# First two token tiles listed from five tiles, routing inside the first product, and stores of x from SyncE's queue

## The chip, the cores and the metric

One core of a Trainium2 chip runs the program. The metric is device time in microseconds (us), median of 3 runs. Line numbers such as L1570 are lines of the kernel before.

## What is computed

```python
attn = local + summary attention of q, k, v      # B=2, H=8, S=768, D=64; window 16, 24 block summaries
x = attn reshaped to (B, S, 512)
for b, s:                                        # expert layer, E=8 experts, F=1024
    e = argmax(x @ w_gate) if s == 0 or gate < 0.5 else expert of token s-1
    out[b, s] = p[e] * (relu(x[b, s] @ w1[e]) @ w2[e])
theta = out @ w_theta                            # third layer
y = w_tok_r @ (out*cos(theta)) + w_tok_i @ (out*sin(theta))
u = out + y;  result = u + relu(u @ w_ch)
```

A token's expert depends on the tokens before it in its batch, so the routing is a running maximum over all tokens. With the inputs that the reference draws, 363 tokens of the first batch go to expert 0, and 269 of them are among its first 640 tokens (five tiles of 128).

## The kernel before

**Attention.** The 1536 tokens are 12 tiles of 128, six to a batch (`TPB = 6`, `NT = 12`). TensorE's turn of one tile g (`tile`, in the block of TensorE) is: scores of tile g+2, transposes of p (the exponentials) of tile g, logits of older tiles, transposes of x of tile g-1, and the product with v (`weigh`). In tiles 0 and 1 the transposes of p stand ahead of the scores. VectorE takes the scores from PSUM (L932), finds the maxima (L938), copies logits (L964) and normalises (`norm`, L959), which writes `x_sb`. ScalarE takes the exponentials (L705) and copies transposed p (L712) and x (L717). GpSimd copies windows of keys (L556) and values (L581 to L585) and the summary rows (`move_rows`, L603) into place, and between them it issues the stores of `x_sb` to the DRAM tensor `xd` (L620), one for each tile. SyncE issues the loads of the first expert's weights, `w1_raw` and `w2_raw`, in four steps each (L485, L488).

**First list.** Expert 0 is the first expert. Which tokens fill its first two slot tiles (`FIRST_TILES = 2`) is found early, from the six tiles of the first batch alone, by the functions `first_...` of VectorE and TensorE (tensors `o_...`, `[P, TPB]` wide). `first_list` ends it: it writes two columns of `slot_list` (L1062), on which GpSimd gathers slot tile 0 from `xd` (`load_first`, L608) into `xin`. The gather of slot tile 1 follows when slot tile 0 has been transposed (`xTf_ready`).

**Full routing.** When the logits of all 12 tiles are there (`logits_back`), VectorE runs one chain of short dependent instructions on tensors `r_...` (L1141 to L1192). TensorE helps it three times: `routing_turn` (L1535), `routing_back` (L1539, L1540) and `routing_ranks` (L1545 to L1547). Then the list of all 21 slot tiles is made by `routing_list` (L1554, twelve matmuls, which need `r_ol` of VectorE and `r_ot` of GpSimd, L641), and the rest of `slot_list` is copied (L1198). VectorE afterwards makes the `table` (L1205 to L1224) that tells each slot tile's weights.

**Products.** A slot tile t is gathered, transposed (`transpose_slots`, L1565), copied by ScalarE and VectorE, multiplied with w1 (`product1`), passed through relu, transposed (`transpose_h`, L1592) and multiplied with w2 (`product2`). The products take float32 as two parts: ScalarE rounds a weight step to its high part `w_h` (L756, L786, L792), VectorE subtracts to get the low part `w_l` (`split_step`, L1095), and three matmuls use them (L1570 to L1572). Only the first product of slot tile 0 (L1621) uses unsplit weights. From slot tile 2 on TensorE needs `table_ready`, since it reads from the table where the weights lie.

**Order.** Each engine runs its instructions in the order in which its block lists them, and semaphores order the engines against each other. The queues that matter here are those of SyncE (hardware DMA) and GpSimd (software DMA).

## Time and profile before

| | us |
|---|---|
| median of 3 runs (lowest, highest) | 424.63 (424.21, 425.11) |
| the profiled execution | 423.96 |
| its span in the trace | 422.2 |
| granted clock of TensorE over the span | 0.999 |

The span is the time between the first and last recorded instruction. The profiled execution takes 1.8 us more than its span, and the median lies 0.67 us above the profiled execution. Times of rows count from the start of the span. A row of a timeline gives start, duration, engine, line, operation, the tensors as out<-in, and how often it stands there; matmuls of one row overlap, so that a row's duration is not the sum of its parts. In brackets stands how long the engine sat idle before it, and for whom.

### The profile page before, as it was taken

The numbers are of one execution on the slowest core, as the hardware profiler recorded it, in microseconds if no ns is written. First come the engines' busy times: TensorE is split into PE (matmuls) and PEld (weight loads), VectorE is DVE, ScalarE is ACT, GpSimd is POOL, SyncE is SP. The second block draws the span as 40 slices with busy tenths as digits, with TensorE's granted clock in tenths as the row PEclk, the third lists the DMA queues.
The fourth block names the chain that finished last, engine by engine and source line by source line (L and its number), as shares of the span: only waits on it lengthen the run. The fifth ranks groups of instructions, "written<-read, shape, count | busy, mean of one in ns | idle before, by whom it ended". The sixth has DMA issues, their size and how long they took to land.

```text
span 422.2 us, 8097 instructions
## 1 busy us (share of the span) xinstructions
PE 409.2 (97%) x2791; PEld 328.6 (78%) x2792; DVE 258.0 (61%) x429; ACT 194.1 (46%) x431; POOL 80.8 (19%) x127
## 2 busy tenths in 40 slices
PE   6889999999999999999999999999999999999996
PEld 3668786468888888888888778888888888888885
DVE  4898998898646327363117595666687646454352
ACT  1698995624647326463247464444433143213110
POOL 3697783221112100121110023200000000000000
PEclk9999999999999999999999999999999999999999
DMA  8995551162989933518130025300000000000012
GB/s 293 412 374 170 185 178 78 51 249 73 380 274 397 367 153 90 208 35 338 50 100 26 0 72 202 100 2 0 0 2 0 26 25 0 27 25 27 25 57 93
DMA packets 17424, 54.50 MB, mean 129 GB/s; under 512 B 2033, under 2 KB 2161, under 8 KB 17137
## 3 DMA queue, kind: packets, MB, share of 16 engines
q1 hardware_dynamic: 12560, 40.98, 27.1%
q0 software_dynamic: 2960, 9.70, 7.0%
q10 hardware_dynamic: 1872, 3.41, 2.1%
q8 instruction: 19, 0.31, 0.3%
q14 instruction: 13, 0.10, 0.1%
HBM read 40.46 MB, written 13.63 MB: 128 GB/s over the span
## 4 chain that ended last, share of the span: by engine, by line
PE 77%; DVE 3%; ACT 3%; DVEq 1%; issue 1%; ACTq 0%; POOL 0%
PE ps L1570 15%; PE ps L1572 14%; PE ps L1571 14%; PE ps L1714 8%; PE ps L1715 8%; PE ps L1716 8%; PE ps L1652 2%; PE ps L1592 2%; PE ps L1621 2%; PE ps L1460 2%; ACT w_h L756 1%; PE ps L1565 1%; DVE w_l L1095 1%; PE ps L1432 1%; DVEq L1102 1%
## 5 line engine op out<-in xcount | busy, mean ns | idle before, releaser
L1714 PE MATMUL ps<-z_h,mix_h 128*128 128x512 f32 x144 | 56.9, 395 | 0.0
L1716 PE MATMUL ps<-z_h,mix_l 128*128 128x512 f32 x144 | 56.1, 390 | 0.0
L1715 PE MATMUL ps<-z_l,mix_h 128*128 128x512 f32 x144 | 56.1, 390 | 0.0
L1570 PE MATMUL ps<-w_h,hT_h 128*128 128x512 f32 x104 | 42.0, 404 | 0.8 <-DVE w_l L1095 0.5
L1095 DVE TENSOR_TENSOR w_l<-w_raw,w_h (+1 forms) x32 | 37.4, 1219 | 8.3 <-ACT w_h L756 8.3
L705 ACT ACTIVATE p<-s,nmax 128x120 f32<-128x120 f32 x96 | 36.5, 384 | 11.1 <-DVE nmax L938 11.1
L1572 PE MATMUL ps<-w_l,hT_h 128*128 128x512 f32 x104 | 40.7, 391 | 0.0
L1571 PE MATMUL ps<-w_h,hT_l 128*128 128x512 f32 x104 | 40.5, 390 | 0.0
L1570 PE MATMUL ps<-w_h,xT_h 128*128 128x512 f32 x96 | 38.4, 400 | 0.0
L1571 PE MATMUL ps<-w_h,xT_l 128*128 128x512 f32 x96 | 37.4, 390 | 0.0
L1572 PE MATMUL ps<-w_l,xT_h 128*128 128x512 f32 x96 | 37.4, 390 | 0.0
L841 ACT ACTIVATE ang_a<-ang_c 128x512 f32<-128x512 f32 x12 | 7.6, 632 | 63.6 <-DVE ang_c L1283 63.6
L1119 DVE TENSOR_TENSOR hT_l<-ps,hT_h 128x512 fp32r<-128x512 f32 x26 | 16.7, 684 | 25.6 <-ACT hT_h L770 25.5
L1716 PEld LDWEIGHTS ps<-z_h,mix_l 128*128 128x128 f32 x144 | 27.0, 188 | 5.8
L1714 PEld LDWEIGHTS ps<-z_h,mix_h 128*128 128x128 f32 x144 | 27.0, 188 | 5.4
L1715 PEld LDWEIGHTS ps<-z_l,mix_h 128*128 128x128 f32 x144 | 27.1, 188 | 5.4
L756 ACT ACTIVATE w_h<-w_raw 128x1024 fp32r<-128x1024 f32 x24 | 23.6, 1051 | 7.8 <-PE ps L1572 5.3
L764 ACT ACTIVATE h_sb<-ps 128x1024 f32<-128x1024 f32 x12 | 12.3, 1024 | 29.2 <-PE ps L1572 29.2
L1113 DVE TENSOR_TENSOR xT_l<-ps,xT_h 128x512 fp32r<-128x512 f32 x12 | 8.3, 689 | 28.3 <-ACT xT_h L760 28.3
L1570 PEld LDWEIGHTS ps<-w_h,hT_h 128*128 128x128 f32 x104 | 19.5, 188 | 5.3 <-DVE w_l L1095 1.3
L1572 PEld LDWEIGHTS ps<-w_l,hT_h 128*128 128x128 f32 x104 | 19.5, 188 | 4.4
L1571 PEld LDWEIGHTS ps<-w_h,hT_l 128*128 128x128 f32 x104 | 19.6, 188 | 3.7
(264 smaller groups left out, 860.2 us busy)
## 6 DMA issues: line engine op xcount, KB each, us to landing
w_raw<-w SPq DMA_DIRECT2D x32, 512.0 KB, 6.2
mix_raw<-mix SPq DMA_DIRECT2D x6, 768.0 KB, 6.0
kfull<-k_full SPq DMA_DIRECT2D x8, 400.0 KB, 6.4
q_all<-q_t SPq DMA_DIRECT2D x6, 512.0 KB, 7.3
vpad<-v_pad SPq DMA_DIRECT2D x4, 768.0 KB, 8.8
xd<-x_sb POOLq DMA_DIRECT2D x12, 256.0 KB, 4.6
ys<-y_sb ACTq DMA_DIRECT2D x12, 256.0 KB, 2.0
out<-o SPq DMA_DIRECT2D x12, 256.0 KB, 2.0
```

What stands on the lines that cost most here:

```text
L705: e = act.activation(p_sb[s][:, n // PAIRS, n % PAIRS, :], s_sb[s][:, n, :], ACT.Exp, bias=nmax[s][:, n:n + 1], accum_out=rsum[s][:, n, 0:1])
L756: act.activation(hi[:, i * SW:(i + 1) * SW, :], raw[:, i * SW:(i + 1) * SW, :], ACT.Copy).then_inc(done, 1)
L764: act.activation(h_sb[:, :].rearrange("p (a n) -> p a n", a=2), ps[:, bank:bank + 2, :], ACT.Relu)\
L1095: dve.tensor_tensor(lo[:, bass.ds(i * SW, SW), :], raw[:, bass.ds(i * SW, SW), :], hi[:, bass.ds(i * SW, SW), :].bitcast(f32), ALU.subtrac ...
L1119: dve.tensor_tensor(hT_l[:, c * 4:c * 4 + 4, :], ps[:, B_HT + c, :].rearrange("p (a k) -> p a k", k=P), hT_h[:, c * 4:c * 4 + 4, :].bitcas ...
L1460: pe.matmul(ps[:, B_Y, :], ident, const[:, 0:DM], start=True, stop=True)
L1570: pe.matmul(ps[:, bank, :], a_h[:, k, :], w_h[:, n, :], start=(k == 0), stop=False)
L1571: pe.matmul(ps[:, bank, :], a_l[:, k, :], w_h[:, n, :], start=False, stop=False)
L1572: return pe.matmul(ps[:, bank, :], a_h[:, k, :], w_l[:, n, :], start=False, stop=(k == last))
L1714: pe.matmul(ps[:, i, :], w_h, zh, start=(jb == 0 and m == 0), stop=False)
L1715: pe.matmul(ps[:, i, :], w_h, zl, start=False, stop=False)
L1716: mm = pe.matmul(ps[:, i, :], w_l, zh, start=False, stop=(jb == TPB - 1 and m == 1))
```

## The change

1. The first list is made from five token tiles instead of six (`FROM = TPB - 1`), and each of its steps stands one token tile earlier or more: `first_logits` and `first_maxima` in tile 7 instead of 8, `first_turn` and `first_scan` in tile 9 instead of 10, `first_back` and `first_choice` in tile 10 instead of 11, `first_rank`, `first_ranks`, `first_lanes` and both `first_list` in tile 11, ahead of the last `weigh` and the last `norm`, instead of after them.
2. In tile 10 VectorE copies both halves of transposed p first of all; in tile 11 ScalarE copies both.
3. In tiles 2 and 3 TensorE transposes p ahead of the scores (it did so in tiles 0 and 1 only).
4. SyncE issues the stores of `x_sb`; GpSimd no longer does. GpSimd moves summary rows 2 and 3 after the key and value windows of its first round.
5. `routing_turn`, `routing_back` and `routing_ranks` stand between the matmuls of the first product of slot tile 0, with one filler matmul (`keep_warm`) instead of six ahead of it; `routing_list` stands ahead of the last quarter of `product1(1)` instead of ahead of all of it; the transposes of slot tile 2 stand in the middle of `product2(0)` instead of ahead of it.
6. Four of the eight low parts of the first expert's weights go to GpSimd (`rest`: steps 2 and 3 of w1, 0 and 1 of w2). They stand between the gather of slot tile 1 and `r_ot`. VectorE makes steps 0 and 1 of w1 ahead of `r_scan`, and steps 2 and 3 of w2. VectorE's copy for slot tile 1 (`xT_copy(1)`) moves into the routing chain.
7. ScalarE rounds two steps of w1 ahead of its last copy of transposed x.

```diff
-WARM, WARM_SUM, WARM_SLOTS = (5, 1), (1, 0), (3, 1, 1, 1)
+WARM, WARM_SUM, WARM_SLOTS = (5, 1), (1, 0), 1
+FROM = TPB - 1
@@ SyncE
+            for g in range(NT):
+                sp.wait_ge(norm_done, g + 1)
+                sp.dma_start(xd[g * P:(g + 1) * P, :], x_sb[:, g, :]).then_inc(x0_saved if g < TPB else x_saved, 16)
@@ GpSimd
             for g in range(NT):
-                pool.wait_ge(norm_done, g + 1)
-                pool.dma_start(xd[g * P:(g + 1) * P, :], x_sb[:, g, :]).then_inc(x0_saved if g < TPB else x_saved, 16)
+                if g == NT - 1:
+                    pool.wait_ge(x0_saved, 16 * TPB)
+                    pool.wait_ge(olist_done, 1)
+                    load_first(0)
...
             load_first(1)
+            def rest(i, raw, hi, lo, hi_done, done):
+                pool.wait_ge(hi_done, i + 1)
+                pool.tensor_tensor(lo[:, i * SW:(i + 1) * SW, :], raw[:, i * SW:(i + 1) * SW, :],
+                                   hi[:, i * SW:(i + 1) * SW, :].bitcast(f32), ALU.subtract).then_inc(done, 1)
+            pool.wait_ge(w1_split, STEPS + STEPS // 2)
+            for i in range(STEPS // 2, STEPS):
+                rest(i, w1_raw, w1_h, w1_l, w1_hi, w1_split)
+            for i in range(STEPS // 2):
+                rest(i, w2_raw, w2_h, w2_l, w2_hi, w2_split)
@@ VectorE, tile
+                if g == NT - 2:
+                    pT_copy(g, 0)
+                    pT_copy(g, 1)
+                if g == NT - 1:
+                    first_ranks()
+                    first_lanes()
                 inverse(g, s)
@@ TensorE, tile
-                if sc and g > 1:
+                if sc and g > SUMMARY_TILES:
                     scores(g + 2, s)
+                if g == NT - 1:
+                    first_rank()
                 transpose_p(g, s, first)
@@ TensorE, first product
+                    if (c, k) == (0, 0):
+                        routing_turn()
+                    if (c, k) == (0, 1):
+                        routing_back()
+                    if (c, k) == (1, 0):
+                        routing_ranks()
+                    if (c, k) == (1, 1):
                         transpose_slots(1)
...
-            routing_list()
-            product1(1, 0)
-            transpose_slots(2)
-            product2(0, 0, first=True)
+            product1(1, 0, middle=routing_list)
+            product2(0, 0, first=True, middle=lambda: transpose_slots(2), at=KF // 2)
```

GpSimd's queue after the last value windows, before the change:

```order
L620 DMA xd<-x_sb 128x512 [waits norm_done] x2
L608 DMA xin<-xd,slot_list 128x512 [waits olist_done,x0_saved]
L608 DMA xin<-xd,slot_list 128x512 [waits xTf_ready]
L641 ISA
L641 TENSOR_TENSOR r_ot<-r_in,const 128x252 [waits tiles_ready]
L651 DMA xin<-xd,slot_list 128x512 [waits xTf_ready,list_done,x_saved]
```

and after it, where the instruction that loads GpSimd's code for such operations (ISA) and four subtractions follow the two gathers:

```order
L612 DMA xin<-xd,slot_list 128x512 [waits olist_done,x0_saved]
L612 DMA xin<-xd,slot_list 128x512 [waits xTf_ready]
L648 ISA
L648 TENSOR_TENSOR w_l<-w_raw,w_h 128x1024 [waits w1_hi,w1_split]
L648 TENSOR_TENSOR w_l<-w_raw,w_h 128x1024 [waits w1_hi]
L648 TENSOR_TENSOR w_l<-w_raw,w_h 128x1024 [waits w2_hi] x2
L657 TENSOR_TENSOR r_ot<-r_in,const 128x252 [waits tiles_ready]
L667 DMA xin<-xd,slot_list 128x512 [waits xTf_ready,list_done,x_saved]
```

So `r_ot` now stands behind four more operations of GpSimd.

TensorE from the gather of slot tile 0 (`xin`) to the routing's ranks, before the change (L1460 are fillers, L1621 is the first product):

```order
L1460 MATMUL ps<-const 128x512 x3
L1535 MATMUL ps<-const,r_v 12x128 [waits v_ready]
L1460 MATMUL ps<-const 128x512
L1539 MATMUL ps<-const,r_scan 128x12 [waits scan_ready]
L1540 MATMUL ps<-const,r_scan 128x12
L1460 MATMUL ps<-const 128x512
L1565 MATMUL ps<-const,xin 128x128 [waits xin_in]
L1565 MATMUL ps<-const,xin 128x128 x3
L1460 MATMUL ps<-const 128x512
L1545 MATMUL ps<-r_oe,tri_b 128x96 [waits cum_ready,onehot_ready]
```

and after it (the first product is L1637):

```order
L1585 MATMUL ps<-const,xin 128x128 x3
L1477 MATMUL ps<-const 128x512
L1637 MATMUL ps<-w_raw,xT_f 128x512 [waits w1_in3,w1_in2,xTf_taken,w1_in1,w1_in0]
L1554 MATMUL ps<-const,r_v 12x128 [waits v_ready]
L1637 MATMUL ps<-w_raw,xT_f 128x512
L1558 MATMUL ps<-const,r_scan 128x12 [waits scan_ready]
L1559 MATMUL ps<-const,r_scan 128x12
L1637 MATMUL ps<-w_raw,xT_f 128x512 x3
L1564 MATMUL ps<-r_oe,tri_b 128x96 [waits cum_ready,onehot_ready]
```

The waits for the routing now stand inside the product instead of ahead of it.

VectorE around its last normalisation (`x_sb`), before the change:

```order
L959 TENSOR_TENSOR x_sb<-ps,rinv 128x512 [waits av_ready]
L964 COPY logitsT_164<-ps 128x128 [waits lg_ready]
L1048 SCALAR_TENSOR_TENSOR o_off<-ps,o_oe 128x6 [waits orank_ready]
L1049 TENSOR_SCALAR o_slot<-o_off 128x6 [waits o_link]
L1050 TENSOR_SCALAR o_tile<-o_slot 128x6 [waits o_link]
L1051 TENSOR_SCALAR o_lane<-o_slot 128x6
L1054 TENSOR_TENSOR o_in<-o_tile,const 128x12 [waits o_link]
L1056 TENSOR_TENSOR o_ot<-o_in,const 128x12 [waits o_link]
L1057 TENSOR_TENSOR o_ol<-o_lane,const 128x768
L964 COPY logitsT_165<-ps 128x128 [waits lg_ready]
L1062 CAST slot_list<-ps 128x2 [waits olist_ready]
```

and after it:

```order
L1079 TENSOR_TENSOR o_ol<-o_lane,const 128x640
L968 TENSOR_REDUCE rsafe<-rsum_158 128x8 [waits exp_done]
L970 RECIPROCAL rinv<-rsafe 128x8 [waits rsafe_done]
L981 COPY logitsT_165<-ps 128x128 [waits lg_ready,rinv_done]
L1084 CAST slot_list<-ps 128x2 [waits olist_ready]
L976 TENSOR_TENSOR x_sb<-ps,rinv 128x512 [waits av_ready]
L981 COPY logitsT_164<-ps 128x128 [waits lg_ready]
L1088 TENSOR_TENSOR w_l<-w_raw,w_h 128x1024 [waits w1_hi]
L981 COPY logitsT_165<-ps 128x128 [waits lg_ready]
```

The whole first list now stands ahead of the last normalisation, and the first low part of w1 between the last two copies of logits.

## Rows read from the trace of the kernel before

**Rows 1.** The page: engines' shares, and the chain that ended last by engine.
```profile
PE 409.2 (97%) x2791; PEld 328.6 (78%) x2792; DVE 258.0 (61%) x429; ACT 194.1 (46%) x431; POOL 80.8 (19%) x127
...
PE 77%; DVE 3%; ACT 3%; DVEq 1%; issue 1%; ACTq 0%; POOL 0%
```

**Rows 2.** Timeline of TensorE in the attention tiles (start, us, what, idle before).
```profile
25.32 1.05 PE L1403 MATMUL ps<-kw,q_all 64*64 64x120 f32 x32 [0.69 <-POOL kw L556]
...
28.77 1.15 PE L1432 MATMUL ps<-v,pT 120*64 120x64 f32 x32 [0.43 <-ACT pT L712]
...
58.18 1.05 PE L1403 MATMUL ps<-kw,q_all 64*64 64x120 f32 x32 [0.43 <-POOL kw L556]
...
65.67 1.15 PE L1432 MATMUL ps<-v,pT 120*64 120x64 f32 x32 [0.85 <-DVE pT L943]
```

**Rows 3.** Timeline of TensorE, the list, h and the product of slot tile 2.
```profile
80.39 5.40 PE L1621 MATMUL ps<-w_raw,xT_f 128*128 128x512 f32 x12
...
89.12 0.45 PE L1554 MATMUL ps<-r_ot,r_ol 128*128 128x21 f16 x12
...
100.95 1.03 PE L1592 MATMUL ps<-const,h_sb 128*128 128x128 f32 x8
101.74 0.48 PE L1570 MATMUL ps<-w_h,xT_h 128*128 128x512 f32 x1
```

**Rows 4.** Timeline of VectorE, the routing chain.
```profile
74.17 0.26 DVE L1141 TENSOR_REDUCE r_m<-ps 128x12 f32<-128x96 f32 x1 [0.26 <-PE ps L1455]
...
75.50 1.22 DVE L1095 TENSOR_TENSOR w_l<-w_raw,w_h 128x1024 fp32r<-128x1024 f32 x1
...
78.75 0.58 DVE L1156 TENSOR_TENSOR r_oe<-r_e,const 128x96 bf16<-128x96 int32 x1
79.37 0.36 DVE L1159 TENSOR_TENSOR_SCAN r_cum<-const,r_oe 128x96 bf16<-128x96 f32 x1
79.64 1.20 DVE L1095 TENSOR_TENSOR w_l<-w_raw,w_h 128x1024 fp32r<-128x1024 f32 x1
...
81.93 0.19 DVE L1170 TENSOR_TENSOR_SCAN r_end<-const,r_al 128x16 f32<-128x16 f32 x1
...
82.43 0.20 DVE L1174 TENSOR_TENSOR r_over<-ps,r_al 128x42 f32<-128x42 f32 x1
...
85.11 2.23 DVE L1192 TENSOR_TENSOR r_ol<-r_lane,const 128x768 f16<-128x768 uint32 x2
```

**Rows 5.** Timeline of GpSimd, gathers and its one two-input operation.
```profile
74.64 1.01 POOL L608 DMA_INDIRECT xin<-xd,slot_list  x1 [2.71 <-DVE slot_list L1062]
79.85 1.85 POOL L608 DMA_INDIRECT xin<-xd,slot_list  x1 [4.20 <-PE ps L1565]
85.27 1.25 POOL L641 TENSOR_TENSOR r_ot<-r_in,const 128x252 f16<-128x252 f32 x1 [3.57 <-DVE r_in L1188]
90.53 1.24 POOL L651 DMA_INDIRECT xin<-xd,slot_list  x1 [4.01 <-DVE slot_list L1198]
```

**Rows 6.** The line of the first two gathers: from issue to landing.
```profile
DMA to landing us min/median/max: 3.4/3.9/4.5
```

**Rows 7.** Timeline of all engines: short VectorE operations beside GpSimd's copies.
```profile
60.33 1.04 POOL L603 COPY v<-v 24x1024 f32<-24x1024 f32 x1
...
62.25 0.61 POOL L581 COPY v<-vpad 64x512 f32<-64x512 f32 x1
62.29 0.59 DVE L1020 TENSOR_TENSOR o_t<-o_lg,o_m 128x6 f32<-128x6 f32 x1
```

**Rows 8.** The line of `r_ol`: durations in ns, least, median and greatest.
```profile
L1192 DVE TENSOR_TENSOR r_ol<-r_lane,const x2: 954/1160/1366, 85.1 to 86.0; 128x768 f16<-128x768 uint32 x2
```

**Rows 9.** The line of `r_ot`, the sequencer's instruction ahead of it.
```profile
L641 POOLq MODIFY_POOL_CONFIG  x2: 47/47/47, 81.7 to 81.7; - x2
```

**Rows 10.** Timeline of VectorE, from slot tile 2's copy to the table's last write.
```profile
96.76 0.69 DVE L1113 TENSOR_TENSOR xT_l<-ps,xT_h 128x512 fp32r<-128x512 f32 x1
...
100.46 0.16 DVE L1224 TENSOR_TENSOR table<-r_tf 1x20 int32<-1x20 f32 x1
```

More of the change, by code:

```diff
@@ L479, in _ @@
             load_v(1)
[L480 to L488 removed]
+            for g in range(NT):
+                sp.wait_ge(norm_done, g + 1)
+                sp.dma_start(xd[g * P:(g + 1) * P, :], x_sb[:, g, :]).then_inc(x0_saved if g < TPB else x_saved, 16)
+                if g == 0:
+                    load_q(2)
+                    sp.dma_start(const[:, C_UT:C_END], const_d[:, C_UT:C_END]).then_inc(rconst_in, 16)
+                elif g <= STEPS:
+                    part = slice((g - 1) * SW, g * SW)
+                    sp.dma_start(w1_raw[:, part, :], w1_d[0, :, part, :]).then_inc(w1_in[g - 1], 16)
+                elif g <= 2 * STEPS:
+                    part = slice((g - STEPS - 1) * SW, (g - STEPS) * SW)
+                    sp.dma_start(w2_raw[:, part, :], w2_d[0, :, part, :]).then_inc(w2_in[g - STEPS - 1], 16)
             sp.wait_ge(logits_back, 1)
@@ L615, in _ @@
             value_window(1)
-            for n in range(1, VB):
-                move_rows(0, n)
+            move_rows(0, 1)
             for g in range(NT):
-                pool.wait_ge(norm_done, g + 1)
-                pool.dma_start(xd[g * P:(g + 1) * P, :], x_sb[:, g, :]).then_inc(x0_saved if g < TPB else x_saved, 16)
+                if g == NT - 1:
+                    pool.wait_ge(x0_saved, 16 * TPB)
+                    pool.wait_ge(olist_done, 1)
+                    load_first(0)
                 if g == TPB:
@@ L630, in _ @@
                     value_window(g + 2)
+                if g == 0:
+                    for n in range(2, VB):
+                        move_rows(0, n)
                 if g == TPB - 2:
@@ L986, in tile @@
                     lg_copy(g - 2)
-                if g == TPB + 2:
+                if g == FROM + 2:
                     first_maxima()
-                if g == NT - 3:
+                if g == FROM + 3:
                     first_other()
+                if g == NT - 2:
+                    first_choice()
                 if g == NT - 1:
-                    first_choice()
+                    first_list()
                 norm(g)
-                if g == TPB + 2:
+                if g == FROM + 2:
                     first_fresh()
-                if g == NT - 3:
+                if g == FROM + 3:
                     first_code()
+                    first_keys()
             linked = [0]
@@ L1193, in _ @@
                                   const[:, C_LANE:C_OWN].unsqueeze(1).broadcast_to([P, NT // 2, P]), ALU.is_equal).then_inc(lanes_ready, 1)
-            w1_step(2)
-            xT_copy(1)
             dve.wait_ge(list_ready, 1)
             dve.tensor_copy(slot_list[:, FIRST_TILES:NS], ps[:, B_R, R_LIST + FIRST_TILES:R_LIST + NS]).then_inc(list_done, 1)
-            w1_step(3)
             hT_copy(0)
-            for i in range(STEPS):
+            dve.wait_ge(w2_split, STEPS + STEPS // 2)
+            for i in range(STEPS // 2, STEPS):
                 split_step(i, i, w2_raw, w2_h, w2_l, w2_hi, w2_split)
@@ L1524, in _ @@
             route_logits(NT - 2)
-            first_rank()
             transpose_x(NT - 1)
@@ L1546, in routing_ranks @@
                 pe.matmul(ps[:, B_R, R_RANK:R_RANK + E * NT], ones_b[:, :], r_cum[:, :, :].rearrange("p e j -> p (e j)"), start=False, stop=True)
-                pe.matmul(ps[:, B_R, R_COUNT:R_COUNT + V], ones_b[:, :], r_cum[:, :, TPB - 1:NT:TPB], start=True, stop=True).then_inc(count_ready, 1)
+                pe.matmul(ps[:, B_R, R_COUNT:R_COUNT + V], ones_b[:, :], r_cum[:, :, TPB - 1:NT:TPB], start=True, stop=True)
+                pe.matmul(ps[:, B_R, R_COUNT + V:R_COUNT + V + 1], ones_b[:, :], r_cum[:, 0, FROM - 1:FROM], start=True, stop=True).then_inc(count_ready, 1)
             def routing_list():
@@ L1572, in product, with product1 @@
                 return pe.matmul(ps[:, bank, :], a_h[:, k, :], w_l[:, n, :], start=False, stop=(k == last))
-            def product1(t, place):
+            def product1(t, place, middle=None):
                 pe.wait_ge(xTf_taken, t + 1)
@@ L1577, in product1 @@
                 for k in range(KD):
+                    if middle and k == KD - 1:
+                        middle()
                     pe.wait_ge(w1_split, place * STEPS + (STEPS + k + 1))
@@ L1593, in transpose_h, with product2 @@
                 mm.then_inc(hT_ready, 1)
-            def product2(t, place, first=False, middle=None, bank=B_Y):
+            def product2(t, place, first=False, middle=None, at=KF // 4, bank=B_Y):
                 if not first and bank == B_Y:
@@ L1598, in product2 @@
                 for k in range(KF):
-                    if middle and k == KF // 4:
+                    if middle and k == at:
                         middle()
```

151 lines of the change are left out of this document (64 added, 87 removed).

## The prediction

> **What bounds the kernel now.** I read the page's shares first, then TensorE's timeline for idle brackets and fillers, then the timelines of VectorE and GpSimd where TensorE waits. TensorE is busy 97% of the span, and 77% of the chain that ended last is its work [rows 1]. From slot tile 2 on (101.74 in [rows 3]) all engines do the same work in the same order in both kernels. So I forecast one number: when that product starts. A shift of it is a shift of the end, as long as the second expert's weights, whose load follows the table, keep pace; they shift with it.
>
> Before that start there are two places to win. In attention TensorE sits idle four times for something that the change moves: 0.69, 0.43, 0.43 and 0.85, together 2.4 us [rows 2]. Between attention and the first product it runs fillers, until 80.39 [rows 3]. The fillers cover a chain: first list, gather, transposes on one side, full routing on the other. After the product the routing goes on beside it, and ends in the twelve matmuls of the list, done at 89.12 + 0.45 = 89.57 [rows 3].
>
> **Attention.** The two waits for keys (0.69, 0.43) end: GpSimd no longer issues stores between its copies. The wait of 0.43 for ScalarE's copy ends too, since transposed p comes ahead of the scores in tiles 2 and 3, and that of 0.85 with the copies of tile 10 put first. Paid back: `first_choice`, the ranks and the lanes (a dozen short operations of VectorE) now stand ahead of the last two normalisations, the last transposes of p wait for `first_rank`, and VectorE, full in tiles 2 and 3, gives no more than half a microsecond there. Bounds are a gain of 0 and of 2.4; working tile by tile with the durations of before I come to 1.1, near the middle. `r_m`, the first step of the full routing, then starts at 74.17 - 1.1 = 73.1 [rows 4]. The slot list is ready some 5 us earlier, the gather of slot tile 0 lands about 73.3, and the first product starts at about 74.6 instead of 80.39. This looks like a gain of 5.8 us.
>
> **The stores.** SyncE's queue only waits for normalisations that it waited for already; 256 KB more on that queue for each tile delay weights that are needed some 20 us later. Cost zero; if that cover fails it is a fraction of a microsecond in the loads. Fewer fillers cost nothing: the clock was granted in full over the idle gaps of before.
>
> **The chain behind the first product.** From `r_m` to the end of `r_v` it is 1.4 us, so `r_v` is done at 74.5, and `w_l` (1.2, [rows 4]) ends at 75.7. GpSimd's second gather started at 79.85 and took 1.85 instead of 1.01 [rows 5], ending 0.86 after the `w_l` that started at 79.64 [rows 4]: VectorE's operation held it up. The same pair meets again here, so the gather ends between 75.7 and 76.5; I take 76.3. Now four subtractions of 1024 elements follow on GpSimd, and they are the crux.
>
> How long is one? The trace has no such operation. Its single-input copy of 1024 elements took 1.04 [rows 7], the lower bound. `r_ot` with two inputs took 1.25 for 252 elements [rows 5], scaled by 1024/252 it is 5.1, the upper bound. But the first `r_ol` took 0.95 and ran until 86.0, the second took 1.37 and so waited 0.41 [rows 8]: `r_ot` itself worked only from 86.0 to 86.5, about 0.5 us. Scaled that is 2.1, and I take it: four make 8.4.
>
> Who waits for them? `o_t`, six elements wide, took 0.59 and ended at 62.88, where the GpSimd copy beside it ended at 62.86 [rows 7]; `r_end`, 16 elements wide and with no GpSimd beside it, took 0.19 [rows 4]. So a VectorE operation that reads two tensors of SBUF waits until GpSimd's operation is over, and GpSimd gets its turn between two of VectorE's, as `r_ot` did between the `r_ol`. The routing chain is made of such operations. While GpSimd has four subtractions of 2.1 us, the chain gets through about one blocked operation for each: `r_oe`, `r_cum` and `r_al` (0.58, 0.36 and about 0.17, together 1.1) between them. So GpSimd is done at 76.3 + 8.4 + 1.1 = 85.8. What is left of the chain then is `r_end` to `r_rest` (81.93 to 82.43, 0.5), the copy for slot tile 1 that was moved in (0.7), `r_over` to the end of `r_ol` (82.43 to 87.34, 4.9) and the last matmuls of the list (0.1). The list is ready at 85.8 + 6.2 = 92.0, where it was 89.57. The four subtractions that VectorE sheds (1.2 each) don't pay for it: two of them stood behind the list, and one of the other two moves ahead to `lg_copy`.
>
> TensorE waits in this stretch. `routing_ranks` needs `r_cum`, which comes near 81.5 while TensorE is there at 79.6; `product1(1)` needs the copy for slot tile 1, at 87.0; the list waits for `r_ol`. TensorE's 5.8 us of lead are gone at the list.
>
> **A rule of the Trainium skill on the size.** `r_ot`'s own 0.5 us for 252 elements is the row [rows 5, 8]. GPSIMD Engine Reference, section 3.1, gives 4497 ns for a two-input operation of 2048 elements, an estimate of 2.25 us for 1024. The sum would be 0.6 us longer by that page. No run so far shows such an operation at this size.
>
> **From the list to slot tile 2's product.** Before, TensorE's own work filled it: 101.74 - 89.57 = 12.2 us, of which 48 matmuls and four transposes took 11.4, or 0.23 for a matmul [rows 3]. Now six matmuls of product1(1), the 24 of product2(0) and twelve transposes stand behind the list, 8.2 us, so another path decides: copy of the list and issue of the gather (89.57 to 90.53, 1.0), landing 3.4 after the issue [rows 6], transposes 0.45, ScalarE's copy 0.6, VectorE's copy 0.7, the table (97.45 to 100.62, 3.2) [rows 5, 10], and TensorE's read of the table's register, which no row isolates: between 0 and 101.74 - 100.62 = 1.1, I take 0.8 since the sequencer must fetch it before it can issue. That is 10.15. VectorE's subtraction of w2 now meets the gather's issue; by the row of 1.85 against 1.01 this costs 0 to 0.9, and I take 0.5: 10.7.
>
> **The sum.** Slot tile 2's product starts at 92.0 + 10.7 = 102.7 instead of 101.74, a loss of 1.0 us. The profiled execution would take 423.96 + 1.0 = 425.0, the median, which lies 0.67 above, 425.6.
>
> **Rivals.**
> *A. GpSimd's subtractions don't hold VectorE up, or much less.* Against it stand the rows of `o_t` and the second `r_ol` [rows 7, 8]; for it, that no row shows a long two-input operation of GpSimd beside a chain of short ones. Then the first product runs from 74.6 for 7.0 us (eight matmuls, six of which took 5.2 [rows 3]) with 1.2 of routing and transposes inside, h takes 1.3, three quarters of product1(1) 18 x 0.23 = 4.1, and with 0.4 for its twelve matmuls the list is ready at 88.6 by TensorE's own pace (VectorE by 87.1). Plus 10.2 makes 98.8, a gain of 2.9: 421.7. It decides from the point where the four together hold the chain up by less than 3.9 us, since a list at 91.0 gives no change. A subtraction of 1.7 us instead of 2.1 lies on the way there, with 424.0.
> *B. GpSimd's code isn't ready.* Ahead of its first two-input operation stands an instruction that changes its configuration, at 81.7 [rows 9], and the operation began 3.57 us later, waiting for VectorE [rows 5]. A load behind it of up to 3.6 us would have been hidden. Now the subtractions follow at once. They would start at 79.9 and hold up a later piece of the chain: GpSimd done near 88.9, the list at 95.0, the end 4.0 us later: 428.6. For it is that nothing in the trace excludes it, against it that no packet of code size on the DMA queues follows the instruction. The Trainium skill has a rule for this (GPSIMD Engine Reference, section 2.1): a first call of freshly loaded code pays 5.95 us. In the trace `r_ot` was over 4.8 us after the instruction, so the trace does not agree with the full figure.
> *C. The first list is short.* If five tiles held fewer than 256 tokens of expert 0, a slot tile more would be needed, about 12 us. The inputs give 269, so this is excluded.
>
> **How the numbers follow.** Forecast (lock at 1.9 to 2.4 us each, attention gaining 0.4 to 1.8): 58%, own range 424.2 to 427.2. A with its neighbours: 22%. B: 12%. Anything else, such as TensorE's clock falling in the new waits: 8%. The range reaches part of the way into A and B: 422.4 to 427.9. A measurement tells 0.2%, 0.85 us, from no change. Faster by more than that is A and the forecast's lower tail: 0.28. Within it lies a quarter: 0.24. Slower takes the forecast's upper half and B: 0.48.
>
> **What would show it.** In the trace of the changed kernel: the gather of slot tile 0 issued near 70; the first product starting near 74.6; four GpSimd rows of about 2.1 us from 76.3; beside them single routing operations of VectorE (`r_oe`, `r_cum`, `r_al`) lasting 1 to 2 us instead of 0.2 to 0.6; idle time of TensorE for `r_cum` and `r_ol`; the list at 92; slot tile 2's product at 102.7 behind the table. The forecast is wrong if those operations keep their durations, if the first subtraction starts 3 us after the gather, or if attention ends more than 2 us earlier.

## The result: 1% slower, in two parts

| | before | after |
|---|---|---|
| median of the executions, us | 424.42 | 428.21 (426.57 to 431.54) |
| ratio, 95% interval | | 1.0095 (1.0072 to 1.0119) |
| the profiled execution, its span | 423.96, 422.2 | 426.57, 424.8 |
| granted clock in it | 0.999 | 0.999 |

The forecast was 425.6, with a range up to 427.9. The profiled executions, both at full clock, lie 2.6 us apart. "After" below is the changed kernel. Its median lies another 1.6 above its profiled execution. The nine executions of after fall in three groups: spans of 424.8 to 425.1 at clocks of 0.995 to 0.999, spans of 426.3 to 426.6 at 0.995 to 0.996, and spans of 428.7 to 429.2 at 0.987 to 0.992. So two questions: where do 2.6 us go at full clock, and why does TensorE's clock fall in many executions? The 2.6 is one pair of executions. By medians the full-clock part is smaller: the changed kernel lies 3.8 us above its kernel before, and 1.7 when its clock is held up (e5).

TensorE of after, timeline (start, us, what, how often, idle before), to be read against [rows 3]:

```profile
76.25 1.10 PE L1637 MATMUL ps<-w_raw,xT_f 128*128 128x512 f32 x2
...
84.56 0.20 PE L1564 MATMUL ps<-r_oe,tri_b 128*128 128x96 bf16 x1 [3.09 <-DVE r_cum L1178]
...
93.23 0.46 PE L1574 MATMUL ps<-r_ot,r_ol 128*128 128x21 f16 x12
...
104.22 0.49 PE L1590 MATMUL ps<-w_h,xT_h 128*128 128x512 f32 x1 [1.97 <-issue]
```

The first product starts 4.1 us earlier than before (80.39). Inside it TensorE waits 3.09 us for `r_cum`. The list is ready at 93.69 (before 89.57), and slot tile 2's product starts at 104.22 (before 101.74): 2.5 us late, about the difference of the spans. From 84.56 to the list TensorE works with a single gap of 0.25 us, and `r_ol` is done at 92.84, 0.4 before TensorE gets to the list: what makes the list late is the wait for `r_cum`, with TensorE's own work behind it. Of the idle 1.97 ahead of the product the profile names no releaser; the last write of the table ended at 103.13, 1.09 earlier. That distance is 1.10 or 1.11 in the traces of e1, e2, e5, e6 and e7 too, which fits a product that waits for the table.

VectorE of after, to be read against [rows 4]:

```profile
74.58 0.26 DVE L1160 TENSOR_REDUCE r_m<-ps 128x12 f32<-128x96 f32 x1 [0.47 <-PE ps L1472]
...
78.95 0.17 DVE L1172 TENSOR_TENSOR r_w<-ps,r_carry 128x12 int32<-128x12 f32 x1
79.16 0.45 DVE L1173 TENSOR_SCALAR r_e<-r_w 128x12 int32<-128x12 int32 x1
79.64 2.67 DVE L1175 TENSOR_TENSOR r_oe<-r_e,const 128x96 bf16<-128x96 int32 x1
82.34 2.06 DVE L1178 TENSOR_TENSOR_SCAN r_cum<-const,r_oe 128x96 bf16<-128x96 f32 x1
...
85.39 1.19 DVE L1186 TENSOR_SCALAR r_al<-r_ti 128x16 int32<-128x16 int32 x1
...
90.60 2.24 DVE L1211 TENSOR_TENSOR r_ol<-r_lane,const 128x768 f16<-128x768 uint32 x2
```

GpSimd of after, to be read against [rows 5]:

```profile
70.81 1.13 POOL L612 DMA_INDIRECT xin<-xd,slot_list  x1 [11.76 <-DVE slot_list L1084]
75.75 0.95 POOL L612 DMA_INDIRECT xin<-xd,slot_list  x1 [3.81 <-PE ps L1585]
77.21 9.34 POOL L648 TENSOR_TENSOR w_l<-w_raw,w_h 128x1024 fp32r<-128x1024 f32 x4 [0.52 <-DVE w_l L1088]
```

The four subtractions take 9.34 us without a gap, 2.335 each, and end at 86.55. If they are equally long, their borders lie at 79.54, 81.88, 84.21 and 86.55. `r_e` ends at 79.61, `r_oe` at 82.31, `r_cum` at 84.40, `r_al` at 86.58: each right behind a border, by 0.03 to 0.43 us, which is no more than its own work. `r_w`, which takes one input from PSUM, keeps its 0.17 in the middle of a subtraction, and so do the three operations on PSUM behind the ranks (L1183 to L1185; 0.17, 0.15 and 0.22, from 84.87 on).

### The profile page after: what moved, and what is told of

Its sections match the earlier page's. It is cut to its first block, busy times and chain, and to the rows that moved or that the text cites. A ratio compares the mean times of both kernels' runs of the same rounds, so it can differ in the third digit from the quotient of the medians.

```text
span 424.8 us, 8082 instructions
## 1 busy us (share of the span) xinstructions
PE 407.6 (96%) x2781; PEld 326.9 (77%) x2782; DVE 257.2 (61%) x424; ACT 194.6 (46%) x432; POOL 81.9 (19%) x119
## 4 chain that ended last, share of the span: by engine, by line
PE 81%; DVE 8%; ACT 4%; DMA 2%; issue 2%; DVEq 1%; POOL 0%; SPq 0%; ACTq 0%; POOLq 0%
PE ps L1590 15%; PE ps L1592 14%; PE ps L1591 14%; PE ps L1734 8%; PE ps L1736 8%; PE ps L1735 8%; PE ps L1672 2%; PE ps L1449 2%; PE ps L1614 2%; PE ps L1420 2%; ACT w_h L772 1%; PE ps L1430 1%; DMA kfull<-k_full 1%; PE ps L1585 1%; DVE s L949 1%
## 5 line engine op out<-in xcount | busy, mean ns | idle before, releaser
L1088 DVE TENSOR_TENSOR w_l<-w_raw,w_h (+1 forms) x28 | 32.7, 1220 | 8.1 <-ACT w_h L772 8.1
```

Source lines behind the costliest of these rows:

```text
L1088: dve.tensor_tensor(lo[:, bass.ds(i * SW, SW), :], raw[:, bass.ds(i * SW, SW), :], hi[:, bass.ds(i * SW, SW), :].bitcast(f32), ALU.subtrac ...
```

## Experiments

Times of the experiments compare with a kernel before of 424.73 (e1 to e4), 424.81 (e5 to e8) and 424.58 (e9 to e12) in the same sets. "Slot tile 2's product" is called the product below.

### e1: the low parts back on VectorE

```diff
@@ GpSimd
-            for i in range(STEPS // 2, STEPS):
-                rest(i, w1_raw, w1_h, w1_l, w1_hi, w1_split)
-            for i in range(STEPS // 2):
-                rest(i, w2_raw, w2_h, w2_l, w2_hi, w2_split)
@@ VectorE, behind r_cum
+            w1_step(2)
@@ VectorE, behind the copy of the list
+            w1_step(3)
@@ VectorE, behind hT_copy(0)
-            for i in range(STEPS // 2, STEPS):
+            for i in range(STEPS):
```

> The changed kernel, but VectorE makes all eight low parts: steps 2 and 3 of w1 behind r_cum and behind the copy of the list, all four of w2 behind hT. GpSimd goes from the second gather straight to r_ot. Theory (GpSimd's subtractions hold VectorE's two-input operations): r_oe, r_cum and r_al fall back to 0.6, 0.4 and 0.2 us (with the subtractions: 2.67, 2.06, 1.19), r_cum ends near 80.2 instead of 84.4, TensorE's wait of 3.09 for it is under 0.5, the list is ready at 88.7 to 89.7 instead of 93.7, slot tile 2's product starts at 99 to 100.5 instead of 104.2, and the profiled execution takes 421 to 423. Rival (the loss comes from the new places of the list and of the transposes behind it): the product stays at 103 to 104 and the time at 425 to 427. For the clock: if TensorE's idle time of 3 us lets the granted clock fall in most executions, it is back at 0.998 or more in all of them, and median and profiled execution lie within 1 us; if the low clock has another reason, it shows 0.987 to 0.996 here too.

Measured: 425.42 (ratio 1.0006, 0.9989 to 1.0023), profiled 427.00. Timeline of VectorE:

```profile
79.09 0.58 DVE L1170 TENSOR_TENSOR r_oe<-r_e,const 128x96 bf16<-128x96 int32 x1
79.71 0.36 DVE L1173 TENSOR_TENSOR_SCAN r_cum<-const,r_oe 128x96 bf16<-128x96 f32 x1
...
81.88 0.17 DVE L1182 TENSOR_SCALAR r_al<-r_ti 128x16 int32<-128x16 int32 x1
```

Timeline of TensorE, the list and what follows:

```profile
89.75 0.46 PE L1570 MATMUL ps<-r_ot,r_ol 128*128 128x21 f16 x12
91.62 0.50 PE L1586 MATMUL ps<-w_h,xT_h 128*128 128x512 f32 x1 [1.40 <-DVE w_l L1083]
...
94.04 0.47 PE L1586 MATMUL ps<-w_h,hT_h 128*128 128x512 f32 x1 [0.79 <-DVE w_l L1083]
...
103.11 0.65 PE L1586 MATMUL ps<-w_h,xT_h 128*128 128x512 f32 x1 [1.98 <-issue]
```

The hold is gone to the hundredth, and the list is ready at 90.21, 3.5 us earlier than in after (0.5 later than expected). But the product gains only 1.1 (expected 4 to 5), and product and time stand where the rival had them (103 to 104, 425 to 427). The rows decide what the time doesn't: the hold is real, and behind it the two waits for low parts and the table show that VectorE's own 1.2 us for each step are the next limit (e6 tests that). So the subtractions on GpSimd hurt, although VectorE did have work to give away. The clock fell behind the idle 1.98 here: the product's first matmul takes 0.65 us (0.49 in after), and the granted clock of the stretch 100 to 105 is 0.83. The eleven other executions have clocks of 0.996 to 1.000, where 0.998 or more was expected in all.

### e2: six fillers in the wait for r_cum

```diff
                     if (c, k) == (1, 0):
+                        keep_warm(6)
                         routing_ranks()
```

> The changed kernel with six filler matmuls (2.8 us by the rows of the first product) ahead of routing_ranks, inside the first product: TensorE works where it waited 3.09 us for r_cum. Nothing else changes. Clock theory: the profiled execution stays at 426 to 427, the granted clock is 0.998 or more in all executions, and the median falls from 428.2 to 426.5 to 427.0. Rival (the low clock has nothing to do with that wait): the clocks stay between 0.987 and 0.999 and the median near 428.

Measured: 429.16, spans 425.5 to 427.0, clock 0.999 or 1.000 in all six executions. I had mis-sized the filler: a `keep_warm` leaves two records, and six took 5.31 us, to 86.14. The ranks came 1.5 us late, and with them the product (105.80). The clock half of the expectation held. The time half (426.5 to 427.0) missed, and since the fillers overran the wait it doesn't tell what the clock costs. Executions of this kernel also spend 2.4 to 3.1 us outside the span, which is part of the median.

### e3: the kernel before without fillers

```diff
-WARM, WARM_SUM, WARM_SLOTS = (5, 1), (1, 0), (3, 1, 1, 1)
+WARM, WARM_SUM, WARM_SLOTS = (5, 1), (1, 0), (0, 0, 0, 0)
```

> The kernel before without its six fillers between the routing's steps and ahead of the first product: TensorE idles some 5.5 of the 6.7 us from 73.7 to 80.4, in three or four stretches. Order and waits are otherwise the same, and the first product can't start earlier, since it waits for the routing. Clock theory: the granted clock falls in most or all executions, mean 0.985 to 0.995, and the time is 425.5 to 429 instead of 424.4. Rival (idle time of this length does nothing to the clock): 424.0 to 424.6 at 0.999.

Measured: 426.71 (ratio 1.0044, 1.0031 to 1.0057), clock 0.991 or 0.992 in all twelve executions. Stretches (start:end, length, busy time of PE, PEld, DVE, ACT, POOL, then the granted clock, the DMA share and GB/s):

```profile
75.00:80.00 5.00, 2.09 (x8) 1.40 (x8) 3.96 (x13) 2.00 (x3) 1.05 (x2) 0.72 0.16 52
80.00:85.00 5.00, 4.86 (x10) 2.23 (x11) 4.55 (x22) 4.11 (x5) 1.91 (x1) 0.60 0.21 54
```

The first product starts at 80.47, where it started before (80.39), and its first twelve records take 7.16 us instead of 5.40. Idle time that costs nothing by itself costs 1.8 us in these records and 2.0 in the median.

### e4: scores first again in tiles 2 and 3

```diff
-                if sc and g > SUMMARY_TILES:
+                if sc and g > 1:
                     scores(g + 2, s)
@@
-                if g <= SUMMARY_TILES:
+                if g <= 1:
                     scores(g + 2, s)
```

> The changed kernel with the scores of TensorE's turns of tiles 2 and 3 ahead of the transposes of p again, as before. The change won 0.9 us in tile 2 (weigh at 27.9 instead of 28.8) and had lost it by the normalisation of tile 3 (35.78 against 35.62). Theory (VectorE is the limit in tiles 2 and 3, so the order there moves nothing but TensorE's waits): norm(3) within 0.3 of 35.8, r_m within 0.3 of 74.58, time within 0.4 of the changed kernel. Rival (the turned order cost something in tile 3, an instruction fetch of TensorE of 0.83 us for one): norm(3) at 35.1 or earlier and r_m 0.5 or more earlier, and the time 0.5 or more lower.

Measured: `x_sb` of tile 3 at 35.83, `r_m` at 74.47 (after 35.78, 74.58). The order in tiles 2 and 3 moves nothing; that half of the expectation held. The time did not: 429.73 (four executions, clocks 0.987 to 0.996). Its profiled execution is what after's was not, one in which the clock fell. TensorE behind the same wait:

```profile
84.44 0.24 PE L1564 MATMUL ps<-r_oe,tri_b 128*128 128x96 bf16 x1 [3.21 <-DVE r_cum L1178]
...
84.65 2.06 PE L1637 MATMUL ps<-w_raw,xT_f 128*128 128x512 f32 x2
86.50 1.06 PE L1585 MATMUL ps<-const,xin 128*128 128x128 f32 x4
...
105.83 0.49 PE L1590 MATMUL ps<-w_h,xT_h 128*128 128x512 f32 x1 [2.05 <-issue]
```

In after the same two matmuls took 1.10 and the transposes 0.60. Ranks at the same time (84.44 and 84.56), product 1.6 us later (105.83 against 104.22): the price of one fall. Four executions can't say whether the order itself makes falls more frequent.

### e5: five fillers inside the two waits

```diff
                     if (c, k) == (1, 0):
+                        keep_warm(3)
                         routing_ranks()
...
             transpose_h(1)
+            keep_warm(2, B_H)
             pe.wait_ge(table_ready, 1)
```

> The changed kernel with three filler matmuls ahead of routing_ranks (0.89 us each by the twelve records of 5.31 us that the six fillers left; six were too many and delayed the ranks by 1.5 us) and two ahead of the wait for the table, where TensorE idles 2.0 us. Both groups fit inside waits. Clock theory (an execution of the changed kernel loses about 1.6 us for each of these two waits after which the clock falls): slot tile 2's product stays at 104.0 to 104.6, the granted clock is 0.998 or more in all executions, their spans lie close together at 424.6 to 425.4, and the median is 426.4 to 427.2. Rival (fillers only replace idle time and the spread has another source): spans from 425 to 429 as without them.

Measured: 426.52 (ratio 1.0033, 1.0017 to 1.0050), clock 0.999 or 1.000 in eleven of twelve executions and 0.996 in one, spans 423.1 to 425.5. Timeline of TensorE with the fillers (L1477):

```profile
81.08 2.74 PE L1477 MATMUL ps<-const 128*128 128x512 f32 x6
84.41 0.20 PE L1564 MATMUL ps<-r_oe,tri_b 128*128 128x96 bf16 x1 [0.59 <-DVE r_cum L1178]
...
102.11 1.88 PE L1477 MATMUL ps<-const 128*128 128x512 f32 x4
104.24 0.49 PE L1590 MATMUL ps<-w_h,xT_h 128*128 128x512 f32 x1 [0.25 <-issue]
```

The product stands where it stood in after (104.22), and the ratio falls from 1.0095 to 1.0033. That is the clock's part, and it is shown apart from the rest: by medians 1.7 us above the kernel before instead of 3.8, so 2.1 us. Two things stay open. The spans spread more than expected (424.6 to 425.4), at full clock. And two falls at 1.6 us make 3.2, while three executions of after have spans some 4 us longer; none of these was traced.

### e6: VectorE reordered, a version faster than both

```diff
@@ e1, and on VectorE
+            dve.tensor_tensor(r_ls[:, :, :], lge, m_b, ALU.subtract).then_inc(lse_ready, 1)
             xT_copy(1)
...
+            w1_step(3)
             dve.wait_ge(list_ready, 1)
...
-            dve.tensor_tensor(r_ls[:, :, :], lge, m_b, ALU.subtract).then_inc(lse_ready, 1)
-            xT_copy(2)
...
             dve.tensor_tensor(table[0:1, T_NEW, 1:NS], ...).then_inc(table_ready, 1)
+            xT_copy(2)
```

> The kernel with all low parts on VectorE, with three moves on VectorE: step 3 of w1 goes ahead of the wait for the list (VectorE idled 1.28 us there, TensorE waited 1.40 for that step afterwards), r_ls goes ahead of the copy for slot tile 1 (0.70 idle there), and the table goes ahead of the copy for slot tile 2. Theory (behind the list VectorE's own work is the limit, 1.2 us for each step and 3.2 for the table): TensorE's waits of 1.40 and 0.79 for low parts are gone or under 0.4, its wait of 1.98 ahead of slot tile 2's product shrinks to under 0.8, the product starts at 100.0 to 100.8 instead of 103.1, and the full-clock span is 420.0 to 421.2, the median 421.8 to 423.2. Rival (the table isn't what the product waits for, but TensorE's register load and instruction fetch): the product stays behind 101.6 with an idle time near 2.

Measured: 422.67 (ratio 0.9950, 0.9933 to 0.9966), spans 420.1 to 421.8, clock 0.999 or 1.000 throughout. Timeline of TensorE:

```profile
89.98 0.46 PE L1570 MATMUL ps<-r_ot,r_ol 128*128 128x21 f16 x12
...
93.14 0.47 PE L1586 MATMUL ps<-w_h,hT_h 128*128 128x512 f32 x1 [1.15 <-DVE w_l L1083]
...
100.66 0.49 PE L1586 MATMUL ps<-w_h,xT_h 128*128 128x512 f32 x1 [0.48 <-DVE xT_l L1130]
```

The product starts 2.4 us earlier than in e1, from a list 0.2 us later. The wait of 1.40 is gone; one of 1.15 for the first low part of w2 is left, more than expected. The profile puts the last wait down to `xT_l`, but the last write of the table ended at 99.56, 1.10 before the product, within 0.01 of after's distance: this fits a product that still waits for the table.

The gain is that of all the parts together. The stores on SyncE alone (e10) reach a ratio of 0.9972, and the intervals of the two ratios overlap.

### e7: two subtractions on GpSimd instead of four

```diff
-            pool.wait_ge(w1_split, STEPS + STEPS // 2)
-            for i in range(STEPS // 2, STEPS):
-                rest(i, w1_raw, w1_h, w1_l, w1_hi, w1_split)
@@ VectorE: w1_step(2) behind r_cum, w1_step(3) behind the copy of the list
```

> The changed kernel with only w2's two low parts on GpSimd; w1's steps 2 and 3 are VectorE's, behind r_cum and behind the list. Theory (each subtraction of 2.33 us on GpSimd holds the chain up by its own length once VectorE has a two-input operation ready): r_cum ends at 81.8 to 82.4 instead of 84.4, r_al has its 0.2 us back, the list is ready at 90.6 to 91.4 instead of 93.7, slot tile 2's product starts at 101.3 to 102.3 instead of 104.2, the profiled execution takes 423.5 to 425. Rival (the cost is a fixed one, such as the first use of the operation): r_cum stays later than 83.5.

Measured: 425.95 (ratio 1.0037, 1.0017 to 1.0057), profiled 425.60. `r_oe` took 2.67, `r_cum` 0.36 and ended at 82.32, 2.1 earlier than in after, as expected: one subtraction less in the way of it. The list was ready at 91.62, also 2.1 earlier than in after. The product began at 103.48, over a microsecond later than expected, behind waits of 1.40 for step 3 of w1 and 2.02 ahead of the product, as in e1.

### e8: the kernel before with the subtractions alone

```diff
@@ GpSimd, between the second gather and r_ot
+            pool.wait_ge(w1_split, STEPS + STEPS // 2)
+            for i in range(STEPS // 2, STEPS):
+                rest(i, w1_raw, w1_h, w1_l, w1_hi, w1_split)
+            for i in range(STEPS // 2):
+                rest(i, w2_raw, w2_h, w2_l, w2_hi, w2_split)
@@ VectorE: w1_step(2), w1_step(3) and steps 0 and 1 of w2 removed
```

> The kernel before with this one part of the change: four low parts on GpSimd between the second gather and r_ot, started by the two of VectorE. Theory: they start at 80.9 right behind VectorE's step 1, take 2.33 each, let one or two held operations through between them and end near 91; r_ot and with it the list are ready at 91.5 to 93 instead of 89.57; behind the list VectorE has 2.4 to 3.6 us less to do but TensorE's own 12.2 us are the limit there; slot tile 2's product starts at 103.7 to 105.2 instead of 101.74 and the time is 426 to 427.5. Rival (it was the order inside the first product that hurt, not the subtractions): time within 0.5 of 424.5.

Measured: 434.59 (ratio 1.0221, 1.0189 to 1.0252), 7 us above the top of the expectation. Timeline of VectorE:

```profile
82.44 9.85 DVE L1179 TENSOR_SCALAR r_al<-r_ti 128x16 int32<-128x16 int32 x1
```

Timeline of GpSimd:

```profile
81.02 1.85 POOL L608 DMA_INDIRECT xin<-xd,slot_list  x1 [4.19 <-PE ps L1575]
82.96 9.29 POOL L643 TENSOR_TENSOR w_l<-w_raw,w_h 128x1024 fp32r<-128x1024 f32 x4
```

Timeline of TensorE, the first half of the list:

```profile
97.16 0.33 PE L1564 MATMUL ps<-r_ot,r_ol 128*128 128x21 f16 x6 [6.71 <-POOL r_ot L652]
```

One 16-element operation of VectorE was held through all four subtractions. It had been issued at 82.44, while GpSimd was still busy with the gather, and was held when the first subtraction began. I had expected one or two operations to be released between the subtractions, and these to start at 80.9.

### e9: the subtractions behind the ranks

```diff
             pool.wait_ge(w1_split, STEPS + STEPS // 2)
+            pool.wait_ge(count_ready, 1)
```

> The changed kernel with one more wait of GpSimd ahead of its four subtractions: for the ranks of TensorE (count_ready), near 81.0. r_oe and r_cum then run free (0.6 and 0.4 us), and the subtractions meet the stretch of the chain that has one two-input operation after the other. In the kernel before with the subtractions alone, r_al was held for 9.85 us, through all four; in the changed kernel r_oe and r_cum were released at the next border between two subtractions. Theory A (a held operation waits for all that GpSimd has queued if it was already held when they started, otherwise until the next border): r_al is issued after the first subtraction has started, so it is released at a border, after 1.5 to 2.5 us, and the next three operations (r_al, r_end, r_base) take the other borders, 2.3 us each. Theory B (r_al's kind, int32 with one input, is held to the end): r_al takes over 8 us. Either way the chain loses nearly the full 9.3 us: GpSimd done near 90.5, the list at 96 to 98, the profiled execution 429 to 432, slower than the changed kernel.

Measured: 432.21, one execution, clock 0.988. Timeline of VectorE:

```profile
82.00 1.95 DVE L1187 TENSOR_SCALAR r_al<-r_ti 128x16 int32<-128x16 int32 x1
83.98 2.26 DVE L1188 TENSOR_TENSOR r_al<-r_al 128x8 int32<-128x8 int32 x1
86.28 2.29 DVE L1189 TENSOR_TENSOR_SCAN r_end<-const,r_al 128x16 f32<-128x16 f32 x1
88.60 2.24 DVE L1190 SCALAR_TENSOR_TENSOR r_base<-r_end,r_al 128x8 f32<-128x8 f32 x1
```

Timeline of GpSimd:

```profile
81.57 9.24 POOL L648 TENSOR_TENSOR w_l<-w_raw,w_h 128x1024 fp32r<-128x1024 f32 x4 [5.03 <-issue]
```

Theory A came out in all four rows, and theory B is refuted: the same `r_al` that was held for 9.85 in e8 is released after 1.95. What sets e8's case apart is that `r_al` was already held when the subtractions began; that is one case, and no run repeats it. Four operations of 0.2 us took 8.74. The list was ready at 99.21, 1.2 us beyond the expected 96 to 98: TensorE waited 5.79 us, and its clock was 0.50 in 90 to 95.

### e10: the stores of x on SyncE, alone

```diff
@@ SyncE
+                sp.dma_start(xd[g * P:(g + 1) * P, :], x_sb[:, g, :]).then_inc(x0_saved if g < TPB else x_saved, 16)
@@ GpSimd
-                pool.dma_start(xd[g * P:(g + 1) * P, :], x_sb[:, g, :]).then_inc(x0_saved if g < TPB else x_saved, 16)
```

> The kernel before with this one part of the change: SyncE stores x, GpSimd doesn't, and GpSimd moves summary rows 2 and 3 later. TensorE's waits of 0.69 and 0.43 us for keys end. Theory (VectorE's work sets the pace of tiles 2 and 3 and again of tiles 8 to 11, so these waits had slack behind them): r_m starts at 73.8 to 74.3 instead of 74.17 and the time is within 0.5 of the kernel before. Rival (the prediction's step: the waits are on the path): r_m at 73.0 to 73.4, the time 0.8 to 1.1 lower.

Measured: 423.42 (ratio 0.9972, 0.9958 to 0.9987), so 1.2 us faster. The time is the rival's, though `r_m` (73.99) stands where the theory had it. In the profiled execution (423.58) the first tile came late: `x_sb` of tile 0 at 21.05 against 20.71 before. Counted from there, `r_m` comes after 52.94 us (before 53.46), and the last matmul 0.7 us sooner. So moving the stores is worth 0.5 us of attention, where the two waits for keys had been 1.1 long. What the median has beyond the trace's 0.7 isn't located.

### e11: memsets instead of subtractions

```diff
-                pool.tensor_tensor(lo[:, i * SW:(i + 1) * SW, :], raw[:, i * SW:(i + 1) * SW, :],
-                                   hi[:, i * SW:(i + 1) * SW, :].bitcast(f32), ALU.subtract).then_inc(done, 1)
+                pool.memset(lo[:, i * SW:(i + 1) * SW, :].bitcast(f32), 0.0).then_inc(done, 1)
```

> The changed kernel in which GpSimd's four subtractions are memsets of the same tiles, so that it writes 1024 elements and reads none; half of the low parts of the first expert's weights are zero, and the output lacks their share. Theory (what holds VectorE is GpSimd's use of SBUF in general, as in the rows of its copies): r_oe or r_cum, whichever meets a memset, still takes 0.5 us or more longer than its 0.58 or 0.36. Rival (only operations that read two tensors, or read at all, hold it): all of them keep 0.58 and 0.36, and r_cum ends near 80.2. The time is below the changed kernel's in both cases, near 422 to 424.

Measured: 423.08, one execution, clock 1.000. This kernel leaves out the values of four low parts, so only its times count. The four memsets took 3.65 us, from 76.61 to 80.26. `r_e` took 0.83, ending at 79.36, where the third memset ended by these numbers; `r_oe` and `r_cum` kept 0.59 and 0.36. So an operation of GpSimd that reads nothing can hold VectorE too. But by the same numbers `r_oe` and most of `r_cum` ran beside the fourth memset and were not held, as the rival had it. The expectation named `r_oe` or `r_cum`; it was `r_e`. What sets `r_e` apart is that it reads one tensor and the other two read two; whether that is the reason, one execution doesn't show. From `r_m` to the end of `r_cum` it is 6.39 us here, 5.54 in e1 and 9.82 in after.

### e12: the table first, in the kernel before

```diff
-            xT_copy(2)
...
             dve.tensor_tensor(table[0:1, T_NEW, 1:NS], ...).then_inc(table_ready, 1)
+            xT_copy(2)
```

> The kernel before with one move on VectorE: the table ahead of the copy for slot tile 2. With the change's early first list and order this move, with step 3 of w1 and r_ls, took the start of slot tile 2's product from 103.1 to 100.66. Theory (in the kernel before TensorE's own work fills the time from the list to that product, so its start doesn't hang on the table): the product starts at 101.4 to 102.0, the time within 0.5 of the kernel before. Rival (the table was on the path there as well): the product starts below 101.2 and the time is 0.6 or more lower.

Measured: 424.60 (ratio 1.0001, 0.9989 to 1.0014), product at 101.66. The move that won 2.4 us together with two others in e6 is worth nothing here, where TensorE's own work fills the time.

## The prediction, step by step

**Attention: this step failed.** Predicted `r_m` at 73.1, measured 74.58, 0.4 later than before instead of 1.1 earlier: 1.5 us. I had taken a value near the middle of 0 to 2.4, and the bound of 0 was itself wrong, since the change puts more of VectorE's work ahead of the last `x_sb`. By the runs: the stores are worth 0.5 (e10), the order in tiles 2 and 3 nothing (e4), and the rest is a loss. From `x_sb` of tile 7 to that of tile 11 the kernel before takes 16.88, e10 16.25 and after 17.15. So what the change does there beyond the stores costs 0.9 us: the moved steps of the first list, the order of the copies in tiles 10 and 11 and ScalarE's earlier roundings; no run parts these. The four waits of [rows 2], 2.4 us together, did go. But up to the last `x_sb` four others came, 1.95 together: one without a named releaser in tile 3, two for VectorE's copies of transposed p, one for `first_rank`:

```profile
33.65 0.41 PE L1466 MATMUL ps<-xaT,wg 128*32 128x128 f32 x4 [0.83 <-issue]
...
57.30 1.15 PE L1449 MATMUL ps<-v,pT 120*64 120x64 f32 x32 [0.58 <-DVE pT L960]
...
61.88 1.15 PE L1449 MATMUL ps<-v,pT 120*64 120x64 f32 x32 [0.26 <-DVE pT L960]
...
67.07 0.17 PE L1493 MATMUL ps<-o_oe,tri_b 128*128 128x5 bf16 x1 [0.28 <-DVE o_cum L1066]
```

The 0.4 itself is no firm number. Traces with before's attention (e3, e8, e12) have `r_m` at 74.08 to 75.33, and those with after's (e1, e2, e5, e6, e7, e9, e11) at 74.00 to 74.66. None is near 73.1. In the stretch from tile 7 to 11 the three of before take 16.87 or 16.88, the seven of after 17.05 to 17.69.

**Gather and first product.** The gather was issued at 70.81 (said: near 70), the first product came 1.65 later than said, about as much as `r_m`. The second gather was not held up this time: it took 0.95 where I had let VectorE's `w_l` stretch it. It had started 0.16 ahead of the `w_l`; before, it started 0.21 behind it and took 1.85.

**The stores.** Costed at zero they were: 0.5 us won in attention and nothing lost (e10).

**The subtractions hold the chain.** Right in place and mechanism. One took 2.335 instead of 2.1, so that they ended at 86.55 instead of 85.8. The Trainium skill's figure (GPSIMD Engine Reference, section 3.1), from which 2.25 was estimated, was nearer than my scaling of `r_ot`; the measurement decides. The 1.1 that I had added for VectorE's operations between them wasn't there, since the four run without a gap. From their end to the list it was 7.1 instead of 6.2. I had the list wait for `r_ol`; it waited for TensorE's own work behind the late ranks, which reached it 0.4 after the end of `r_ol`. From `r_m` to the list it was 19.1 us in all, forecast 18.9. That these agree is in part luck: 0.6 less to the first subtraction, 0.9 more in the four, 1.1 less between them and 0.9 more behind them cancel. My condition was too narrow: `r_e` and `r_al`, which read one tensor of SBUF, were held too.

**From the list to the product.** Forecast 10.7, measured 10.53, behind the table as said. The 0.5 for a gather's issue held up by VectorE wasn't there (from list to issue it was 0.97), and the read of the table's register took 1.09 instead of 0.8.

**The clock: this step failed too.** "Fewer fillers cost nothing" rested on idle times of at most 0.85 us. My own forecast of a wait of 1.9 us and more inside the product, and a product that waits for the table, should have ended that argument. The falling clock had a part of a share of 8% and no price. A fall takes 1.6 us (e4), and with fillers of the right length 2.1 us of the median's loss are gone (e5).

**The sum.** Product 2.5 us late instead of 1.0: the profiled execution 426.57 instead of 425.0, nearly all of it attention's 1.5. Median minus profiled execution 1.64 instead of 0.67: 1.0, which is the clock, since the profiled execution was one without a fall. Together the miss of 2.6.

**Rivals.** A (no hold) is refuted by the rows of `r_oe`, `r_cum` and `r_al`. Even e1, where nothing holds the chain, had its product at 103.11 and not at 98.8, but there VectorE has the steps to do. B (code not ready) is refuted: the first subtraction starts at 77.21, 0.08 behind the `w_l` that it waited for (75.91 + 1.22) and 0.5 behind the sequencer's instruction:

```profile
L648 POOL TENSOR_TENSOR w_l<-w_raw,w_h x4: 2341/2362/2388, 77.2 to 84.2; 128x1024 fp32r<-128x1024 f32 x4
L648 POOLq MODIFY_POOL_CONFIG  x2: 37/37/37, 76.7 to 76.7; - x2
```

The rule of the Trainium skill on a first call of freshly loaded code (GPSIMD Engine Reference, section 2.1) did not show here: no 5.95 us fit into 0.5.

## What to carry to other kernels

An idle second engine is no free capacity while the first runs a chain of tiny dependent operations: each of them can wait for one whole long operation of the other, so put long GpSimd work beside VectorE's PSUM reads or its waits, and price it by its full length in a dense stretch. VectorE was short of time here, but what helped was order: with the low parts back on it the loss of 1% was gone (e1), and three moves of its own steps made that -0.5% (e6). The stores on SyncE alone, in the kernel before, give -0.3% (e10). And whoever moves a wait into a product must carry the fillers along, cut to the length of the wait.

## What the runs showed of the hardware

- A GpSimd subtraction of two SBUF tensors of 128x1024 float32 takes 2.34 us; VectorE does the same in 1.2 (1.22 in [rows 4]). The memset of that size takes 0.91 (3.65 for four).
- A held VectorE operation is released at the next border between two GpSimd operations if it was issued inside one (after, e7, e9). In the one case in which it was already held as the queue of subtractions began, it stayed held through all four (e8, 9.85 us). Why is open. Memsets held `r_e`, which reads one tensor, and let `r_oe` and `r_cum` run, which read two (e11, one execution).
- TensorE's first product behind the table starts 1.09 to 1.11 us after the table's last write, in the traces of after, e1, e2, e5, e6 and e7.
- TensorE's granted clock falls to its lower level after some waits and not after others of the same length. After 3.09 us idle it stayed at 1.00 in the profiled execution of after, and after 3.21 it fell in that of e4 (0.73 in 85 to 90). After 1.98 it fell in e1 (0.83 in 100 to 105), after 2.05 in e4 it stayed (1.00 in 105 to 110). The two levels are 1.2 and 2.4 GHz; at the lower one a filler-sized pair of matmuls takes 2.06 instead of 1.10. In e3, with 1.58 and 1.18 us idle close together, it fell in all twelve executions.
